# Expert slots of a routed layer: second products three slots behind the first, second buffers for x, h, turned h and y, and weight loads issued apart

## What is computed

```python
B, S, D, E, F = (4, 576, 512, 8, 1024)
logits = np.einsum('bsd,de->bse', x, w_gate)
local_gate = 1.0 / (1.0 + np.exp(-np.einsum('bsd,de->bse', x, w_local).squeeze(-1)))
for b in range(B):
    prev_e = -1
    for s in range(S):
        fresh_e = int(np.argmax(logits[b, s]))
        if s == 0 or local_gate[b, s] < 0.5:
            e = fresh_e
        else:
            e = prev_e if prev_e >= 0 else fresh_e
        prev_e = e
        ...
        h = np.maximum(x[b, s] @ w1[e], 0.0)
        out[b, s] = p[e] * (h @ w2[e])
```

## Time and profile before

| | us |
|---|---|
| median of 3 runs | 746.09 (745.82 to 746.37) |
| profiled execution | 742.61 |
| its span | 740.8 |
| PE, PEld busy | 718.6, 609.1 |
| DVE, ACT, POOL busy | 462.8, 321.4, 328.2 |

### The profile page before, as it was taken

One profiled execution on the slowest core, in us unless ns is written; L12 is line 12 of the kernel. 1 busy time (PEld: TensorE's weight loads), 2 busy tenths in 40 slices (PEclk: granted clock), 3 DMA queues, 4 the chain that ended last, 5 costly groups with the idle time before them and its releaser, 6 DMA issues.

```text
span 740.8 us, 14655 instructions
## 1 busy us (share of the span) xinstructions
PE 718.6 (97%) x4795; PEld 609.1 (82%) x4795; DVE 462.8 (62%) x1090; ACT 321.4 (43%) x634; POOL 328.2 (44%) x442
## 2 busy tenths in 40 slices
PE   7999999999989998999999999999999999999998
PEld 5888887888877876888787787887899989889986
DVE  5777878878776447666564665665399446536610
ACT  5777878878430023040312403200488335436610
POOL 7759788887337249081909718230421100000000
PEclk9999999999999999999999999999999999999999
DMA  8888889894076876677687777731521100000011
GB/s 171 197 230 212 224 224 226 216 232 121 17 216 184 260 247 218 212 246 253 199 281 256 245 242 226 228 128 44 142 65 30 46 33 15 29 30 15 29 42 58
DMA packets 115691, 116.49 MB, mean 157 GB/s; under 512 B 63884, under 2 KB 84644, under 8 KB 115620
## 3 DMA queue, kind: packets, MB, share of 16 engines
q1 hardware_dynamic: 95092, 69.59, 33.3%
q10 hardware_dynamic: 17056, 34.69, 13.8%
q0 software_dynamic: 3472, 11.28, 5.6%
HBM read 87.66 MB, written 27.86 MB: 156 GB/s over the span
## 4 chain that ended last, share of the span: by engine, by line
PE 64%; DMA 5%; DVE 2%; issue 2%; SPq 0%; POOL 0%; ACT 0%; POOLq 0%; DVEq 0%; ACTq 0%
PE row_bank L1360 17%; PE wide_bank L1343 16%; PE wide_bank L1655 14%; PE row_bank L1693 13%; DMA h_turn<-h_sb 2%; DMA x_slots<-h_turn 2%; PE bank L1309 1%; PE bank L1624 1%; DMA y_tok<-y_sorted,place_i 1%; DMA x_slots<-x_rows,token_of 0%; SPq L1233 0%; DMA y_sorted<-y_sb 0%; PE wide_bank L28 0%; PE bank L1644 0%; POOL y_tok L1597 0%
## 5 line engine op out<-in xcount | busy, mean ns | idle before, releaser
L913 POOL TENSOR_TENSOR ring<-raw_w,ring 128x2048 fp32r<-128x2048 f32 x28 | 128.3, 4607 | 110.8 <-ACT ring L903 110.8
L1360 PE MATMUL row_bank<-ring,h_tr 128*128 x600 | 144.7, 397 | 7.3 <-issue 4.0
L1343 PE MATMUL wide_bank<-ring,xs_tr 128*128 x600 | 142.8, 394 | 3.0 <-issue 2.3
L903 ACT ACTIVATE ring<-raw_w 128x2048 fp32r<-128x2048 f32 x30 | 55.8, 1908 | 203.1 <-DMA raw_w<-in_moe_w_dram 160.3
L1360 PEld LDWEIGHTS row_bank<-ring,h_tr 128*128 128x128 f32 x600 | 111.9, 190 | 31.6 <-issue 9.0
L1343 PEld LDWEIGHTS wide_bank<-ring,xs_tr 128*128 128x128 f32 x600 | 113.4, 190 | 27.3 <-issue 4.1
L1655 PE MATMUL wide_bank<-x_tr,ring 128*128 128x288 f32 x768 | 107.4, 297 | 0.0
L1655 PEld LDWEIGHTS wide_bank<-x_tr,ring 128*128 128x128 f32 x768 | 103.2, 188 | 1.1 <-issue 0.4
L1693 PE MATMUL row_bank<-ring,g_tr 128*128 128x512 f32 x432 | 100.2, 390 | 0.0
L1693 PEld LDWEIGHTS row_bank<-ring,g_tr 128*128 128x128 f32 x432 | 80.5, 188 | 16.1
L692 ACT ACTIVATE prob<-score,row_min 128x128 f32<-128x128 f32 (+2 forms) x144 | 83.4, 580 | 18.4 <-DVE row_min L555 15.4
(11 more groups left out here) (242 smaller groups left out, 989.9 us busy)
## 6 DMA issues: line engine op xcount, KB each, us to landing
raw_w<-in_moe_w_dram ACTq DMA_DIRECT2D x12, 2048.0 KB, 11.5
h_turn<-h_sb SPq DMA_DIRECT2D x22, 512.0 KB, 3.2
x_slots<-h_turn SPq DMA_DIRECT2D x88, 128.0 KB, 3.0
ncum_row<-cum_rows SPq DMA_DIRECT2D x15, 512.0 KB, 5.7
y_sorted<-y_sb SPq DMA_DIRECT2D x26, 256.0 KB, 3.0
raw_w<-in_moe_w_dram SPq DMA_DIRECT2D x12, 512.0 KB, 4.0
ncum_tail<-cum_rows SPq DMA_DIRECT2D x32, 144.0 KB, 4.5
out_dram<-out_sb ACTq DMA_DIRECT2D x18, 256.0 KB, 2.0
```

The lines of the kernel that those rows point to most:

```text
L903: nc.scalar.activation(high, whole, ACT.Copy).then_inc(high_ready, 1)
L913: nc.gpsimd.tensor_tensor(low, whole, high.bitcast(F32), ALU.subtract).then_inc(low_ready, 1)
L1343: last = nc.tensor.matmul(h_bank[:, half, :], xs_tr[:, a, kb, :], ring[:, bass.ds(n, 1), b, at:at + FH].rearrange("p a c -> p (a c)"), sta ...
L1360: last = nc.tensor.matmul(y_bank[:, :], h_tr[:, a, kb, :], ring[:, bass.ds(n, 1), 2 + b, kb * D:(kb + 1) * D].rearrange("p a c -> p (a c)" ...
```

## The change

TensorE's loop becomes `turn_x(s+1)`, `hidden(s)`, `output(s-3)`. Slot 2 too is turned by TensorE (`BY_PE = 3`). Odd slots get buffers of their own: `xs_other` for x (on the memory of `last_at`), `h_other` for h from slot 5 on and `h_tr_other` for turned h from slot 9 on (both on used parts of `x_slots`), and `bank[1]` for y. `h_exchange` is parted into `h_write` and `h_read`, both still on SyncE's queue, and `y_store(s-4)` stands ahead of `h_write(s)`. VectorE's program is rewritten to fit, with x moved two slots ahead. On ScalarE the second matrix is loaded after the next first matrix has been copied. `turn_last` comes after `output(23)`. Two semaphores that nothing waited for are gone.

```diff
-    BY_PE = 2
+    h_bank, ht_bank, x_bank, y_banks = wide_bank[0], wide_bank[1], bank[0], (row_bank[0], bank[1])
+    BY_PE = 3
+    BEHIND = 3
+    h_other = x_slots[:, 4:6, :].rearrange("p s d -> p (s d)")
+    H_OTHER = 5
+    h_tr_other = nc.alloc_sbuf_tensor_at("h_tr_other", [P, 2, KF, P], F32R, offset=address(x_slots) + 6 * 4 * D)
+    HT_OTHER = 9
...
+    def outputs_until_free(s):
+        if s < HT_OTHER:
+            return s
+        return s - 1 if s != HT_OTHER else 0
...
+    xs_other = nc.alloc_sbuf_tensor_at("xs_other", [P, 2, KD, P], F32R, offset=address(last_at))
+    xs_both = (xs_tr, xs_other)
...
-        def h_exchange(s):
+        def h_write(s):
             n, i = s % 2, s - BY_PE
             sp.wait_ge(h_ready, 2 * s + 2)
-            above(sp, h_back, 16 * QUARTERS * i)
-            sp.dma_start(h_turn[n], h_sb[:, :]).then_inc(h_out, 16)
+            above(sp, h_back[n], 16 * QUARTERS * (i // 2))
+            sp.dma_start(h_turn[n], h_of(s)).then_inc(h_out, 16)
+
+        def h_read(s):
+            n, i = s % 2, s - BY_PE
             sp.wait_ge(h_out, 16 * (i + 1))
-            if i >= 2:
-                sp.wait_ge(h_blocks, 2 * i - 2)
+            above(sp, h_blocks, 2 * i - 2)
...
         y_store(0)
-        h_exchange(2)
         y_store(1)
-        h_exchange(3)
-        h_exchange(4)
-        for s in range(2, SLOTS - 1):
+        for s in range(BY_PE, SLOTS - 1):
+            if s == 5:
+                y_store(2)
+            elif s >= 7:
+                y_store(s - BEHIND - 1)
+            h_write(s)
+            h_read(s)
+        for s in range(SLOTS - 1 - BEHIND - 1, SLOTS - 1):
             y_store(s)
-            if s + 3 < SLOTS - 1:
-                h_exchange(s + 3)
...
         for e in range(2, E):
             first_matrix(e + 1)
+            high_parts(act, (e + 1) % 2, (e + 1) // 2, 0)
             second_matrix(e)
-            high_parts(act, (e + 1) % 2, (e + 1) // 2, 0)
             high_parts(act, e % 2, e // 2, 1)
...
-            above(pe, y_ready, s)
+            above(pe, y_ready, s - 1)
...
         hidden(0, (1,), n)
         n = weights_of(1, 0)
         turn_h(0)
+        turn_x(2)
         hidden(1, loaded=n)
-        turn_x(2)
         output(0)
         turn_h(1)
+        turn_x(3)
         hidden(2)
-        turn_x(3)
         output(1)
-        hidden(3)
-        turn_x(4)
-        for s in range(4, SLOTS - 1):
+        turn_h(2)
+        for s in range(BY_PE, SLOTS - 1):
+            turn_x(s + 1)
             hidden(s)
-            turn_x(s + 1)
-            output(s - 2)
-
+            if s == 4:
+                output(2)
+            elif s >= 6:
+                output(s - BEHIND)
         s = SLOTS - 1
         hidden(s, (0,))
+        output(s - 3)
         output(s - 2)
+        output(s - 1)
         turn_last()
-        output(s - 1)
...
         def move_x(s):
             dve.wait_ge(xs_turned, s + 1)
-            above(dve, h_done, 2 * s)
+            above(dve, h_done, 2 * s - 2)
...
         def relu(s, halves=range(2)):
             for half in halves:
                 dve.wait_ge(h_done, 2 * s + (1 + half))
-                if s > BY_PE:
-                    dve.wait_ge(h_out, 16 * (s - BY_PE))
-                else:
-                    above(dve, ht_turned, 2 * s + (half - 1))
+                if s > H_OTHER:
+                    dve.wait_ge(h_out, 16 * (s - 1 - BY_PE))
+                elif s == BY_PE + 1:
+                    dve.wait_ge(h_out, 16)
+                elif s <= BY_PE:
+                    dve.wait_ge(ht_turned, 2 * s if s == BY_PE else 2 * s + (half - 1))
...
-        for s in range(1, SLOTS - 1):
-            if s >= 4:
-                h_turned(s - 2)
-                move_h_blocks(s - 2)
-            if s == 3 or s > 4:
-                move_y(s - 3 if s > 4 else 1)
-            relu(s)
-            move_x(s + 1)
-            if s == 1:
-                move_y(0)
-                move_h(1)
...
+        move_x(4)
+        relu(3)
+        move_x(5)
+        relu(4)
+        move_x(6)
+        move_y(2)
+        h_turned(3)
+        move_h_blocks(3)
+        relu(5)
+        move_x(7)
+        for s in range(6, SLOTS - 1):
+            if s > 6:
+                move_y(s - BEHIND - 1)
+                move_h_blocks(s - BEHIND)
             relu(s)
+            h_turned(s - 2)
+            if s + 2 < SLOTS:
+                move_x(s + 2)
```

More of the change, by code:

```diff
@@ L1193, in mixture, with h_of, ht_of @@
     y_sb = sb("y_sb", [P, D], where=region)
-    h_bank, ht_bank, x_bank, y_bank = wide_bank[0], wide_bank[1], bank[0], row_bank[0]
-    BY_PE = 2
+    h_bank, ht_bank, x_bank, y_banks = wide_bank[0], wide_bank[1], bank[0], (row_bank[0], bank[1])
+    BY_PE = 3
+    BEHIND = 3
     h_swapped = [x_slots[:, 2 * n:2 * n + 2, :].rearrange("p s d -> p (s d)") for n in range(2)]
-    h_out, h_back, h_blocks, y_begun = sem("h_out"), sem("h_back"), sem("h_blocks"), sem("y_begun")
+    h_other = x_slots[:, 4:6, :].rearrange("p s d -> p (s d)")
+    H_OTHER = 5
+    h_tr_other = nc.alloc_sbuf_tensor_at("h_tr_other", [P, 2, KF, P], F32R, offset=address(x_slots) + 6 * 4 * D)
+    HT_OTHER = 9
+    h_out, h_back, h_blocks = sem("h_out"), [sem(f"h_back{n}") for n in range(2)], sem("h_blocks")
+    def h_of(s):
+        return h_other if s % 2 and s >= H_OTHER else h_sb[:, :]
+    def ht_of(s):
+        return h_tr_other if s % 2 and s >= HT_OTHER else h_tr
+    def outputs_until_free(s):
+        if s < HT_OTHER:
+            return s
+        return s - 1 if s != HT_OTHER else 0
     HK = KF // 2
@@ L1296, in pool_experts, with quarters_of_half @@
         low_parts(pool, E, 1)
[L1298 to L1301 removed]
+    def quarters_of_half(s, half):
+        by_quarter = h_of(s).rearrange("p (g k c) -> p g k c", g=QUARTERS, k=KF)
+        return by_quarter[:, :, half * HK:(half + 1) * HK, :].rearrange("p g k c -> p k g c")
     def tensor_experts(pe):
@@ L1342, in hidden @@
                     for a, b in PARTS:
-                        last = nc.tensor.matmul(h_bank[:, half, :], xs_tr[:, a, kb, :],
+                        last = nc.tensor.matmul(h_bank[:, half, :], xs_both[s % 2][:, a, kb, :],
                                                 ring[:, bass.ds(n, 1), b, at:at + FH].rearrange("p a c -> p (a c)"),
@@ L1363, in output @@
                                             stop=kb == KF - 1 and (a, b) == PARTS[-1])
-                if kb == HK - 1 and s == SLOTS - 3:
-                    last.then_inc(y_begun, 1)
             if KF - 1 in blocks:
@@ L1512, in vector_experts @@
         dve.wait_ge(last_zeroed, 16)
-        for s in range(1, SLOTS - 1):
-            if s >= 4:
-                h_turned(s - 2)
-                move_h_blocks(s - 2)
-            if s == 3 or s > 4:
-                move_y(s - 3 if s > 4 else 1)
-            relu(s)
-            move_x(s + 1)
-            if s == 1:
-                move_y(0)
-                move_h(1)
-        h_turned(SLOTS - 3)
-        move_h_blocks(SLOTS - 3)
-        move_y(SLOTS - 4)
-        relu(SLOTS - 1, (0,))
+        relu(1)
+        move_x(2)
+        move_y(0)
+        move_h(1)
+        relu(2)
+        move_x(3)
+        move_y(1)
+        move_h(2)
+        move_x(4)
[12 more added lines that the diff above has]
+                move_h_blocks(s - BEHIND)
+            relu(s)
+            h_turned(s - 2)
+            if s + 2 < SLOTS:
+                move_x(s + 2)
+        s = SLOTS - 1
+        move_y(s - BEHIND - 1)
+        move_h_blocks(s - BEHIND)
+        relu(s, (0,))
         V.tensor_scalar(last_row[:, :], place_i[:, 0:TB], -1.0, float(LAST), ALU.mult, ALU.add).then_inc(last_placed, 1)
@@ L1533, in vector_experts @@
                 .then_inc(last_made, 1)
+        h_turned(SLOTS - 3)
+        move_h_blocks(SLOTS - 3)
+        move_y(SLOTS - 4)
         h_turned(SLOTS - 2)
-        move_h_blocks(SLOTS - 2, (0,))
+        move_h_blocks(SLOTS - 2)
         move_y(SLOTS - 3)
-        move_h_blocks(SLOTS - 2, (1,))
         move_y(SLOTS - 2)
@@ L1661, in tensor_block @@
         pe.wait_ge(last_ready, 2)
+        pe.wait_ge(y_ready, SLOTS - 1)
         for t in range(3):
```

43 lines of the change are left out of this document (19 added, 24 removed).

## The result

| | before | after |
|---|---|---|
| median, runs (lowest to highest) | 743.63, 6 (739.72 to 746.37) | 732.25, 6 (729.72 to 733.19) |
| profiled execution, its span | 742.61, 740.8 | 730.58, 728.8 |
| after / before | | 0.9844, interval 0.9804 to 0.9884 |

Against these three alone the gain by the medians is 8.9, less than the 12.03 between the two profiled executions. The forecast was 734.2 (731.5 to 739.0), and 730.7 for the profiled execution, which took 730.58.

A forecast was written before the change was run, and what follows sets the result against it. TensorE, busy 97%, bounds the kernel, so only its idle time can be won. 14.55-0.79-1.05-0.3-0.5 = 11.9 us saved: 742.61 to 730.7 profiled, median 746.09 to 734.2, range 731.5 to 739.

The forecast's parts named there:

- Items 2, 3, 4: TensorE's losses to go: wait at slot 3's second product 3.53, its slowed clock 1.33, slots 6 to 23 4.74 us.
- item 4: Slots 6 to 23: 4.74 us lost in five places, h's trip through DRAM being too long beside two weight loads.
- Item 1: Slot 4's first product: 2.06 us lost, x split late because slot 3's relu waited for slot 2's h write.
- Items 5, 6: The slots' end, y's one bank emptied late: 0.96 and 0.55 us; slot 1's first product: 0.57 us.
- Item 7: After the last product TensorE waits for the gathered y: 0.81 us with the restart, counted whole as gain.
- Cost (a): One more turning of h by TensorE, eight transposes: 0.79 us.
- Cost (b): Lead-in: slot 5's relu comes late on VectorE, a new TensorE wait before slot 6 of 1.05 us.
- Cost (c): Second weight matrices asked for later, tightest at expert 6 with cover nil: 0.3 us, ends 0 and 3.3.
- Cost (d): SyncE: y stores behind h's waiting reads delay VectorE's splits: 0.5 us over the run, ends 0 and 7.8.
- The rival of late second matrices: Weight loads landing at 14.5 us give all back; at 15, 17.4 lost, 12.2 saved, 751.3; chance 0.05.
- The 12.4: Saving in us if an h write beside loads took about twice its 3.0 us, making cost (d) nil.
- The carry to the median: The 11.9 us saving applied to the runs' median, 746.09, 3.5 above the profiled execution: 734.2.

The follow-up runs named there:

- these three: Three runs of the kernel before, unchanged, made beside the changed kernel: 741.15, 741.44 and 739.72 us.
- the later chips: Three chips used for the experiments; the changed kernel run again there took 748.80 us against 757.43 for the kernel before.
- the small loads: Kernel before, with weight loads from expert 2 on, their copies and low parts cut to a quarter: 748.91 us against 756.61.
- the one-bank kernel: Changed kernel with one bank for y instead of two: 755.03 us, one run.
- spacing alone: Kernel before with only ScalarE's order changed, the second matrix loaded after the next first one is copied: 760.77 us, ratio 1.0057.
- changed, h twice: Changed kernel with each h written to DRAM twice, the second write waiting for the first: 780.68 us.
- before, h twice: Kernel before with each h written to DRAM twice, the second write waiting for the first: 797.78 us.

## The prediction against the traces

**What bounded it: right.** Idle time of TensorE was all there was to win: 11.54 of 12.03 are waits gone between 229 and 512, less the two costs.

**Items 2, 3, 4: right in place and size, and item 4 in cause.** None of the waits is left, the clock is 1.00 in 280 to 300, and 16 slots take 16 x 11.36. VectorE's waits for `x_slots<-h_turn`, 43.4 us before, are in no row after. Item 4's cause is shown by the small loads. For items 2 and 3 it is read from the trace alone: they didn't come back on the later chips.

**Item 1: right in place and size, wrong in cause.** I put the 1.82 down to the 3.71 that slot 3's relu waited for the write of slot 2's h. With small loads that wait was gone and the 1.82 stayed, and in the kernel before the second half of the relu waited last for TensorE. What removed it is the second half of my reason, `move_x(4)` ahead of the relu, and not that the relu waits for no transfer. The number came out right by luck.

**Items 5, 6: right in place and size.** The trace after has none of these waits. For item 5 the one-bank kernel brought them back, and in the changed order, with three second products in a row, their price is 4.8 and not 1.5.

**Item 7: mis-sized.** I counted 0.81 whole; 0.45 came, and on the later chips none of it can be told (4.47 before, 4.54 changed). The wait is gone in every trace of the changed kernel, but other gaps take its place ahead of the third layer's product.

**Cost (a): right,** 0.87 (252.86 to 253.73) for 0.79. **Cost (b): right,** 1.08 (6.99 less 5.91) for 1.05, and by the chain described. Its sum is off by a tenth or two: the terms given end the lead-in at 270.51, or 270.87 with the turns of x 2 counted, not at 270.75, and the product after these would want its bank at 276.78 or 277.14. The trace has 271.02, and 277.29 for the bank. VectorE's timeline after:

```profile
271.66 0.69 DVE L1461 CAST xs_tr<-bank 128x512 fp32r<-128x512 f32 x1 [5.19 <-PE bank L1330]
...
272.99 0.68 DVE L1523 COPY y_sb<-row_bank 128x512 f32<-128x512 f32 x1
273.59 1.31 DVE L1469 STREAM_TRANSPOSE wide_bank<-x_slots 128x512 f32<-128x512 f32 x2
274.81 0.67 DVE L1479 CAST h_tr<-wide_bank 128x512 fp32r<-128x512 f32 x1
...
277.44 1.28 DVE L1495 TENSOR_SCALAR x_slots<-wide_bank 128x512 f32<-128x512 f32 x2
```

The experiment that takes the relu's half out of this row takes the wait with it, so the cause is shown, not only argued.

**Cost (c): mis-sized, by a wrong step.** I took 0.3, with nil cover at expert 6, because I let the second load leave only after both copies of ScalarE. ScalarE's rows after say otherwise:

```profile
329.60 0.38 ACTq L891 DMA_DIRECT2D raw_w<-in_moe_w_dram  x1
340.83 1.92 ACT L903 ACTIVATE ring<-raw_w 128x2048 fp32r<-128x2048 f32 x1 [17.15 <-DMA raw_w<-in_moe_w_dram]
341.38 0.40 ACTq L891 DMA_DIRECT2D raw_w<-in_moe_w_dram  x1
342.65 1.90 ACT L903 ACTIVATE ring<-raw_w 128x2048 fp32r<-128x2048 f32 x1
...
403.21 0.40 ACTq L891 DMA_DIRECT2D raw_w<-in_moe_w_dram  x1
414.03 3.72 ACT L903 ACTIVATE ring<-raw_w 128x2048 fp32r<-128x2048 f32 x2 [11.04 <-DMA raw_w<-in_moe_w_dram]
```

It leaves 0.55 us into the first copy, some 3.2 us earlier, so the two loads of a pair are mostly 10.4 to 11.9 us apart and not some 15. For expert 6 that brought the pair before to an end sooner: the load of expert 7's first matrix left at 387.90 and not at 393.4. Expert 6's second matrix itself left at 403.21, behind slot 13's second product and both copies; it had landed at 414.03; POOL had its low parts at 425.2, and 431.63 was the time at which they were wanted. The cost is 0 and the cover 6.4 us. The rival of late second matrices needed landings of 14.5; the longest after was 13.2.

**Cost (d): nil here, but the mechanism is real.** I took 0.5 of 7.8. VectorE was late twice, and neither reached TensorE:

```profile
349.44 0.69 DVE L1523 COPY y_sb<-row_bank 128x512 f32<-128x512 f32 x1 [1.19 <-DMA y_sorted<-y_sb]
...
439.97 0.69 DVE L1523 COPY y_sb<-row_bank 128x512 f32<-128x512 f32 x1 [0.84 <-DMA y_sorted<-y_sb]
```

In another execution it reached it with 1.71, and it is the first thing to give way when h takes longer (34.0 us of waits with each h written twice). As to writes of h beside a load: one issued at 330.32, 0.7 us behind a load, let the reads go only at 338.90, 8.6 us on; 9.4 had been taken from the earlier trace rows. So the estimate made from the rule of the Trainium skill ("DMA: Bandwidth & Descriptors", "Queues, rings and completion order"), twice the lone 3.0, is not what these writes took; the row decides, as the sum had it. Whether the turns by packet themselves hold, no run here shows. The 12.4 that it gave would have been 0.4 off where 11.9 was 0.1 off.

**Sum.** 14.55 less 0.36 for item 7, 0.87 and 1.08 give 12.24; measured 12.03. Of the 0.2 left, 0.14 stand ahead of slot 1, where slot 0's turns of h begin at 227.94 and not at 227.80; so slot 1's product starts no earlier though item 6's wait is gone and four turns have moved ahead of it. The errors work against each other: 0.8 too much for (c) and (d), 0.36 too much hoped for from item 7. So the forecast is better than its steps, and part of its nearness is luck.

**The carry to the median** was weak: I added 3.5 for runs above the profiled one. Later runs of before lay at 739.7 to 741.4, below its profiled 742.61, so the 3.5 were not a fixed distance between a profiled execution and the median. Why the first three were slower stays open.

## What to carry to other kernels

When an exchange through DRAM is late by a little beside large transfers, give its consumer one more iteration of distance before touching the transfers: here the new order took out the waits, nearly whatever the order of the loads, and spacing the loads without it made things slower. No run parts the distance of one more slot from the second buffers for x, h and turned h, so how little of the change would have done is not shown. Then look at what shares the queue with the exchange: with each h written twice the next limit was the queue's time per iteration and not the trip. And before putting a consumer's wait down to the longest idle time upstream, look at which wait ended last: here 3.71 us of VectorE's idle time cost TensorE nothing. What a second buffer is worth shows in the prologue and epilogue too: the second y bank earned nothing in 17 slots and some 5 us at the end.

## What the runs showed of the chip

**An issue runs ahead of the copies on its engine.** A DMA that stands behind two ACTIVATEs in ScalarE's program was issued 0.55 us after the first of them began and 1.27 before the second (340.83, 341.38 and 342.65 above). The trace doesn't say why.

**A 512 KB write issued just behind a 2 MB load takes nearly as long as the load.** Alone, h is written and its reads let go in 2.6 us (260.58 to 263.21 after). In the trace after, the writes issued 0.6 to 0.7 behind a load took 8.2 to 9.0, where loads land in 9.8 to 13.2; in the kernel before slot 10's took 9.4. One issued 5.6 behind a load took 6.4 (403.92 above, the load at 398.37). With a quarter of each load no transfer of h took over 5.9.

**The price of a wait.** Products behind waits of 1.96, 3.04 and 3.29 us took 7.40, 7.35 and 7.06 by the profile, where 5.7 is usual. Behind 1.71 one took 5.71, behind 1.82 three took 5.7 and one 7.36, and behind 1.81 one 7.35. But behind 1.99 one took 5.75 (spacing alone, 307.19), behind 2.77 one 5.76 (changed, h twice, 476.66), and behind 2.83 one 5.74 (before, h twice, 277.23). So the idle time alone doesn't tell whether the clock falls, and a wait of some 2 us may cost nearly 4 or only itself.

**TensorE starves in some executions while POOL gathers.** On the three later chips the trace of every kernel, changed or not, showed this between some 242 and 257 us, and the first two traces don't; in the changed kernel:

```profile
246.38 0.39 PE L1381 MATMUL row_bank<-ring,h_tr 128*128 x1 [1.70 <-issue]
248.48 0.59 PE L1381 MATMUL row_bank<-ring,h_tr 128*128 x1 [1.71 <-issue]
...
257.14 7.70 PE L1364 MATMUL wide_bank<-ring,xs_tr 128*128 x24 [0.43 <-issue]
```

and the clock, third from the end, here and in the same stretch of the first trace:

```profile
245.00:255.00 10.00, 3.09 (x10) 1.80 (x10) 1.50 (x3) 0.00 (x0) 4.08 (x5) 0.64 0.69 159
```

```profile
245.00:255.00 10.00, 10.00 (x52) 8.45 (x51) 4.51 (x8) 0.00 (x0) 1.89 (x2) 1.00 0.88 214
```

Single matmuls stand up to 2.1 us apart, and the profile names nothing that they wait for. POOL's 25 gathers run from 213.8 to 250.3 here and from 213.9 to 247.4 in the first trace of the changed kernel, nearly all of them 0.95 us long in both. Slot 0's first product is late here too, at 223.46 against 220.31. Slot 2's first product begins at 241.86 there; elsewhere at 252.9 to 256.2 in kernels of the old order (four traces) and at 254.3 to 259.0 in those of the new (eight). So the changed order may lose 2 to 3 us there, which would be what is missing in 8.6 against 12. Against it stands that the medians of the first runs, those made beside each other, differ by 8.9 as well. The two ranges overlap, no run was made that moves the gathers or the turns against each other, and the cause stays open; that the chip makes the difference isn't shown either, since no kernel has a trace both with and without it on one chip.
